# Attention pairs spread over three steps, with turned weights between a tile's input-side products

## The reference, cut to what matters

```python
scores = scale * q @ k.T                      # B=4, H=8, S=576, D=64, scale 1/8
scores = where(causal, -1e9, scores)
a = softmax(scores); local = a @ v
phi = where(q > 0, q, exp(q) - 1) + 1
mem_out = (phi @ M_prev) / (phi @ z_prev + 1e-6)
attn = g * mem_out + (1 - g) * local          # g = sigmoid(beta), one for each head
x = attn as 2304 tokens x 512
h = x @ w_in                                  # 512 x 1024
solu = h * softmax(h); ln = layernorm(solu) * g_ln
x = ln @ w_out                                # 1024 x 512
out = (sigmoid(x @ w_gate) * (x @ w_val)) @ w_out2    # d_ff 1536
```

## Time and profile before

| | |
|---|---|
| median of 3 runs | 964.6 us (963.66 to 966.36) |
| profiled execution | 962.04 us |
| its span | 960.3 us |
| TensorE busy | 907.2 us, 94% |
| VectorE, ScalarE, GpSimd busy | 408.5, 329.8, 183.5 us |
| mean granted TensorE clock | 0.979 |

### The profile page before, as it was taken

How to read it: one execution, slowest core, us unless ns; L and a number is a source line. 1 busy time by engine, 2 the same in 40 slices (tenths; PEclk the granted TensorE clock), 3 DMA queues, 4 the chain that set the end, 5 groups by cost and what they waited for, 6 DMA issues and landing times.

```text
span 960.3 us, 15231 instructions
## 1 busy us (share of the span) xinstructions
PE 907.2 (94%) x5584; PEld 749.3 (78%) x5584; DVE 408.5 (43%) x972; ACT 329.8 (34%) x740; POOL 183.5 (19%) x144
## 2 busy tenths in 40 slices
PE   5787789999999999999799999999999999999997
PEld 2555557777777777878699989989998998998997
DVE  5666776666766676354414422122112112112112
ACT  3455545545554555345524211121112112112111
POOL 4344322222222120125407410010001001001000
PEclk9889999999999999999999999999999999999999
DMA  5131111111111100400305000000000000000000
GB/s 155 49 127 41 51 40 38 31 33 38 38 38 38 38 26 14 132 1 1 99 1 165 0 33 1 1 18 15 0 0 33 0 0 33 0 0 33 0 0 33
DMA packets 36786, 33.51 MB, mean 35 GB/s; under 512 B 5776, under 2 KB 27280, under 8 KB 36752
## 3 DMA queue, kind: packets, MB, share of 16 engines
q1 hardware_dynamic: 36752, 33.06, 11.6%
HBM read 28.33 MB, written 4.72 MB: 34 GB/s over the span
## 4 chain that ended last, share of the span: by engine, by line
PE 87%; DVE 5%; issue 2%; POOL 2%; ACT 1%; DMA 1%; POOLq 0%; ACTq 0%; SPq 0%; DVEq 0%
PE m_bk L1066 8%; PE s_bk L1089 6%; PE tt_bk L1174 5%; PE s_bk L1176 5%; PE s_bk L1174 5%; PE s_bk L1175 5%; PE tt_bk L1176 5%; PE tt_bk L1175 5%; PE o_bk L1007 5%; PE tt_bk L999 4%; PE s_bk L953 4%; PE o_bk L1089 4%; PE m_bk L1191 3%; PE m_bk L1190 3%; PE m_bk L1189 3%; PE s_bk L1066 2%
## 5 line engine op out<-in xcount | busy, mean ns | idle before, releaser
L886 DVE TENSOR_TENSOR gv<-gv,s_bk 128x384 f32<-128x384 f32 x71 | 39.4, 554 | 289.4 <-PE s_bk L1176 289.4
L530 ACT ACTIVATE p_nat<-s_bk,negmax 128x512 f32<-128x512 f32 (+2 forms) x144 | 77.9, 548 | 94.9 <-DVE negmax L729 94.8
L597 ACT ACTIVATE gv<-tt_bk 128x384 f32<-128x384 f32 x70 | 34.5, 492 | 206.7 <-PE tt_bk L1176 206.7
L1174 PE MATMUL tt_bk<-x_hi,w_hi 128*128 128x384 f32 x280 | 94.7, 338 | 8.2 <-POOL x_lo L492 8.2
L1174 PE MATMUL s_bk<-x_hi,w_hi 128*128 128x384 f32 x288 | 96.3, 334 | 0.0
L1176 PE MATMUL s_bk<-x_hi,w_lo 128*128 128x384 f32 x288 | 96.2, 334 | 0.0
L1175 PE MATMUL s_bk<-x_lo,w_hi 128*128 128x384 f32 x288 | 96.2, 334 | 0.0
L1176 PE MATMUL tt_bk<-x_hi,w_lo 128*128 128x384 f32 x280 | 94.3, 337 | 0.0
L1175 PE MATMUL tt_bk<-x_lo,w_hi 128*128 128x384 f32 x280 | 94.0, 336 | 0.0
L604 ACT CAST gv_hi<-gv 128x384 fp32r<-128x384 f32 x72 | 36.9, 513 | 158.0 <-PE m_bk L1191 135.9
L729 DVE TENSOR_REDUCE negmax<-s_bk 128x1 f32<-128x512 f32 (+2 forms) x144 | 67.4, 515 | 51.0 <-PE s_bk L953 42.7
(11 more groups left out here) (144 smaller groups left out, 1846.6 us busy)
## 6 DMA issues: line engine op xcount, KB each, us to landing
qkT<-in_q SPq DMA_DIRECT2D x16, 288.0 KB, 2.8
qkT<-in_k SPq DMA_DIRECT2D x16, 288.0 KB, 2.8
out<-o_sb SPq DMA_DIRECT2D x18, 256.0 KB, 2.0
v_raw<-in_v SPq DMA_DIRECT2D x16, 256.0 KB, 2.7
w_raw<-in_moe_w_gate SPq DMA_DIRECT2D x12, 256.0 KB, 4.5
w_raw<-in_moe_w_val SPq DMA_DIRECT2D x12, 256.0 KB, 4.9
w_raw<-in_moe_w_out SPq DMA_DIRECT2D x12, 256.0 KB, 6.0
xT<-in_moe_w_in SPq DMA_DIRECT2D x1, 2048.0 KB, 8.5
```

Source lines behind the costliest of these rows:

```text
L530: nc.scalar.activation(dst, s_tile(tile), ACT.Exp, bias=negmax[:, n:n + 1], accum_out=den[:, n:n + 1]).then_inc(exp_ok, 1)
L1174: mm(o, w3_hi[f][:, a], x2_hi[:, d, :], start=d == 0, stop=False)
```

## The change

A pair now takes three steps: its scores and exponentials in step g, the rest of its normalization, its memory output and its turned weights in step g + 1, its weighted values in step g + 2. Turned weights stand between the blocks of the tile's input-side products, and the output products follow in two blocks around the tail tile's scores. `M0` becomes 6, so the last tile of the stage is in a seventeenth step without scores. The mask products go: VectorE adds a float32 mask to the scores, scales by -1/8, writes the sum to `p_nat` (now two buffers) and takes the minimum in one instruction; ScalarE exponentiates in place. q and k get second buffers and are loaded one step ahead; `qs` and `qmin` go. ScalarE makes `qrelu`, VectorE the feature (`feature`); GpSimd keeps only splits and the power. ScalarE copies five fills, VectorE two. The weighted values of the tail go to a bank of their own (`m_bk[0]`), in one function `weighted` that is `weighted_main` followed by `weighted_tail`, with the memory's five transposes first. Loops over steps are unrolled. Of new functions the whole is shown; the old functions of the same names are taken out.

```diff
-    ACT_FILLS = [n for n in range(NF) if n % 2 == 0]
-    DVE_FILLS = [n for n in range(NF) if n % 2 == 1]
+    ACT_FILLS = [0, 2, 4, 5, 6]
+    DVE_FILLS = [1, 3]
...
-    M0 = HP + 1
+    M0 = HP + 2
...
-    T_END = LAST - M0
+    T_END = PAIRS - M0
...
-        W1_AT = {0: (0, 1), 1: (2, 3)}
-        W2_AT = {2: (0, 1, 2), 3: (3, 4, 5), 4: (6, 7)}
+        W1_AT = {1: (0, 1), 2: (2, 3)}
+        W2_AT = {4: (0, 1), 5: (2, 3), 6: (4, 5, 6, 7)}
...
+            def step(g):
+                if g < LAST:
+                    wait(sp, s_ready, NU * g)
+                    wait(sp, qexp_ok, g)
+                    wait(sp, qrelu_ok, g)
+                    sp.wait_ge(q_in, 16 * g + 16)
+                    sp.wait_ge(k_in, 16 * g + 16)
+                    load_q(g + 1)
+                    load_k(g + 1)
+                if g > 1:
+                    sp.wait_ge(o_ready, 2 * g - 2)
+                    load_v(g - 1)
+                if 0 < g < PAIRS:
+                    sp.wait_ge(mem_ready, 2 * g)
+                    load_mz(g)
...
+            def step(g):
+                for c in W1_AT.get(g, ()):
+                    split_w1(c)
+                for f in W2_AT.get(g, ()):
+                    split_w2(f)
+                if g >= M0:
+                    rstd(g - M0)
+                if g >= M0 - 1:
+                    split_x(g - M0 + 1)
...
+            def feature_relu(g):
+                act.wait_ge(q_in, 16 * g + 16)
+                wait(act, phi_ok, g)
+                nc.scalar.activation(qrelu[:, :], qkT[:, g % 2, 0, :], ACT.Relu).then_inc(qrelu_ok, 1)
...
+            def exp_tile(g, n):
+                tile = order[n]
+                unit = [tile in u for u in UNITS].index(True)
+                act.wait_ge(max_ok, NU * g + unit + 1)
+                nc.scalar.activation(p_tile(g, tile), p_tile(g, tile), ACT.Exp, bias=negmax[:, n:n + 1], scale=-1.0,
+                                     accum_out=den[:, n:n + 1]).then_inc(exp_ok, 1)
...
+            def early_step(g):
+                exp_tile(g, 0)
+                exp_tile(g, 1)
+                if g > 1:
+                    keep_both(g - 2)
+                for n in range(2, 6):
+                    exp_tile(g, n)
+                if g:
+                    keep_pt(g - 1, 0)
+                    keep_pt(g - 1, 2)
+                exp_tile(g, 6)
+                exp_tile(g, 7)
+                if g:
+                    keep_pt(g - 1, 4)
+                    keep_pt(g - 1, 5)
+                    keep_pt(g - 1, 6)
+                feature_relu(g + 1)
+                exp_tile(g, 8)
+                feature_exp(g + 1)
+                for c in W1_AT.get(g, ()):
+                    split_w1(c)
+                for f in W2_AT.get(g, ()):
+                    split_w2(f)
...
+            def step(g, t):
+                if g < PAIRS:
+                    exp_tile(g, 0)
+                    exp_tile(g, 1)
+                if t:
+                    moe_ln(t - 1)
+                keep_both(g - 2)
+                if g < PAIRS:
+                    for n in range(2, 6):
+                        exp_tile(g, n)
+                keep_pt(g - 1, 0)
+                if g < PAIRS:
+                    exp_tile(g, 6)
+                    exp_tile(g, 7)
+                if g < LAST:
+                    feature_relu(g + 1)
+                keep_pt(g - 1, 2)
+                keep_pt(g - 1, 4)
+                keep_pt(g - 1, 5)
+                keep_pt(g - 1, 6)
+                moe_exp(t)
+                if g < PAIRS:
+                    exp_tile(g, 8)
+                moe_square(t)
+                for f in W2_AT.get(g, ()):
+                    split_w2(f)
+                moe_x(t + 1, x_done(t + 1))
+                if g < LAST:
+                    feature_exp(g + 1)
+                if t:
+                    moe_y(t - 1)
...
+            def unit_max(g, n):
+                if n == 0:
+                    wait(dve, pt_filled, NF * (g - 1))
+                dve.wait_ge(mask_ok, 3)
+                dve.wait_ge(s_ready, NU * g + n + 1)
+                for tile in UNITS[n]:
+                    c = order.index(tile)
+                    w = keys(tile)
+                    to, m = p_tile(g, tile), mask[:, FULL * P - min(w, FULL * P):FULL * P]
+                    if tile == TAIL_TILE:
+                        to = to.rearrange("p (a n) -> p a n", a=2)
+                        m = mask_tail[:, :].rearrange("p (a n) -> p a n", a=2)
+                    last = nc.vector.tensor_tensor_reduce(out=to, in0=s_tile(tile), in1=m, scale=-SCALE, scalar=3.0e38,
+                                                          op0=ALU.add, op1=ALU.min, accum_out=negmax[:, c:c + 1])
+                last.then_inc(max_ok, 1)
...
+            def feature(g):
+                dve.wait_ge(qrelu_ok, g + 1)
+                dve.wait_ge(qexp_ok, g + 1)
+                wait(dve, mem_ready, 2 * g)
+                nc.vector.scalar_tensor_tensor(out=phi[:, 0:S], in0=qexp[:, :], scalar=1.0, in1=qrelu[:, :], op0=ALU.min,
+                                               op1=ALU.add).then_inc(phi_ok, 1)
...
+            def early_step(g):
+                unit_max(g, 0)
+                unit_max(g, 1)
+                if g:
+                    normalize(g - 1, 1)
+                    normalize(g - 1, 2)
+                unit_max(g, 2)
+                unit_max(g, 3)
+                if g:
+                    scale_memory(g - 1, 0)
+                    scale_memory(g - 1, 1)
+                    keep_pt(g - 1, 1)
+                unit_max(g, 4)
+                unit_max(g, 5)
+                if g:
+                    keep_pt(g - 1, 3)
+                feature(g)
+                unit_max(g, 6)
+                normalize(g, 0)
+                for f in W2_AT.get(g, ()):
+                    scale_w2(f)
...
+            def step(g, t):
+                if g < PAIRS:
+                    unit_max(g, 0)
+                    unit_max(g, 1)
+                if t > 1:
+                    moe_store_x(t - 2)
+                normalize(g - 1, 1)
+                if t:
+                    moe_ln_low(t - 1)
+                normalize(g - 1, 2)
+                if g < PAIRS:
+                    unit_max(g, 2)
+                    unit_max(g, 3)
+                scale_memory(g - 1, 0)
+                scale_memory(g - 1, 1)
+                keep_pt(g - 1, 1)
+                if g < PAIRS:
+                    unit_max(g, 4)
+                    unit_max(g, 5)
+                keep_pt(g - 1, 3)
+                if g < PAIRS:
+                    feature(g)
+                    normalize(g, 0)
+                moe_max(t)
+                moe_rows(t)
+                moe_stats(t)
+                if g < PAIRS:
+                    unit_max(g, 6)
+                for f in W2_AT.get(g, ()):
+                    scale_w2(f)
+                moe_var(t)
+                moe_norm(t)
...
-            def score_mask(tile):
-                n = keys(tile)
-                mm(s_tile(tile)[:, n - P:n], ident_b[:, :], mask_t[:, :], start=True, stop=False, skip_group_check=True)
...
+            def copied(g, n):
+                if n in ACT_FILLS:
+                    pe.wait_ge(pt_act_ok, NA * g + ACT_FILLS.index(n) + 1)
+                else:
+                    pe.wait_ge(pt_dve_ok, ND * g + DVE_FILLS.index(n) + 1)
...
+            def early_step(g):
+                scores(g, 0)
+                if g > 1:
+                    weighted(g - 2)
+                scores(g, 1)
+                if g:
+                    memory(g - 1, None)
+                scores(g, 2)
+                if g:
+                    for n in range(5):
+                        turn_p(g - 1, n)
+                scores(g, 3)
+                if g:
+                    turn_p(g - 1, 5)
+                    turn_p(g - 1, 6)
...
+            def step(g, t):
+                if g < PAIRS:
+                    scores(g, 0)
+                if t > 1:
+                    moe_out_t(t - 2)
+                if t:
+                    pe.wait_ge(pt_act_ok, NA * (g - 1))
+                    pe.wait_ge(pt_dve_ok, ND * (g - 1))
+                    moe_transpose(t - 1)
+                weighted(g - 2)
+                wait(pe, yt_ok, t - 1)
+                if g < PAIRS:
+                    scores(g, 1)
+                memory(g - 1, t)
+                pe.wait_ge(x_ok, 2 * (g - 1))
+                wait(pe, u_ok, t)
+                moe_hidden(t, 0, 8)
+                turn_p(g - 1, 0)
+                turn_p(g - 1, 1)
+                moe_hidden(t, 8, 12)
+                if g < PAIRS:
+                    scores(g, 2)
+                moe_hidden(t, 12, 16)
+                turn_p(g - 1, 2)
+                turn_p(g - 1, 3)
+                moe_hidden(t, 16, 20)
+                turn_p(g - 1, 4)
+                turn_p(g - 1, 5)
+                moe_hidden(t, 20, 24)
+                turn_p(g - 1, 6)
+                if t:
+                    if g < PAIRS:
```

(92 more changed lines are left out.)

280 lines of the change are left out of this document (74 added, 206 removed).

## The result

The changed kernel takes **995.5 us** (median of 4 runs, 993.24 to 996.86), the kernel before 964.3 us beside it (4 runs, 963.66 to 966.36): a ratio of 1.0319, with a 95% interval of 1.0296 to 1.0341. It is slower, as forecast, but by 31 us where I had 8.4; the time lies outside my range of 955 to 988.

A forecast was written before the change was run, and what follows sets the result against it. TensorE fills the 25.45 us steady step, while waits set early steps. Tile 0 came 8.3 us sooner, but nine steps grew to 27.7 us, putting tile 11 8.2 us later: 973 us forecast, range 955 to 988.

The forecast's parts named there:

- Sign and bound: Whole kernel: slower, chance 0.70, because added waits make a steady step 27.7 us although TensorE's own work shrinks.
- TensorE's own sum: Steady step: TensorE alone would need 24.2 us instead of 25.45, with the mask products and some interruptions gone.
- (a): Steady step, first fill of turned weights: TensorE waits 0.2 us for the second half of the scaled memory.
- (b): Steady step, fifth fill: TensorE waits 1.84 us for ScalarE's copy of the third fill, queued behind relu and feature.
- (c): Steady step, the tile's transposes: TensorE waits 1.42 us for VectorE's scaling, which runs beside GpSimd's split of x.
- The maxima as products with a reduction: VectorE's score maxima: the new form costs nothing, at most 0.1 us each; 1.22 us against 1.22 for 1,024 columns.
- The early step: Steps before the steady stage: VectorE sets 14.5 us a step, plus 0.8 for the clock; step 6 begins near 91 us.
- From tile 0 to tile 9: Steady stage between those tiles' transposes: nine steps of 27.7 us less 1.8, from 124.5 to 372.0 us.
- The clock rival: Stretches of waits and transposes drop TensorE's clock in most steps, about 1.7 us each, 15 us in all: 988 us; chance 0.15.
- The larger early gain: Early steps overlap better and take 13.3 us, so six steps give 12 us more: 961 us; chance 0.13.
- The rival without waits: Steady steps without (b) and (c) take 24.4 us, ending 28 us before the forecast: 945 us; chance 0.12.

The follow-up runs named there:

- The first two experiments: Each against the changed kernel: ScalarE's relu moved behind its copies of turned weights, 975.49 us; the square moved ahead of the tail tile's exponential, 977.86 us.
- The fourth experiment: Changed kernel with GpSimd's weight splits delayed to the next step, behind its third score unit: 982.01 us, 1.0184 of the kernel before.
- the kernel with all edits: Changed kernel with relu late, square first, output rows before the next x, GpSimd's weight splits timed and its power first: 940.67 us, 0.9770 of the kernel before.
- the fifth: Changed kernel with delayed GpSimd weight splits, and tile 0's power and next x split ahead of the weight blocks: 980.19 us, 1.0172 of the kernel before.
- the second experiment: Changed kernel with ScalarE squaring the tile's rows before the tail tile's exponential: 977.86 us, 1.0141 of the kernel before.

## Why the prediction was off

**Sign and bound: right.** TensorE's own work did shrink, and the waits that the new order puts in took more than it gave. But the 31 us are not those of my sum: the steady waits are, the early part's are not.

**TensorE's own sum: right in kind, a little small.** I had 24.2 us a step. With nearly all waits gone it is 24.4 (24.67 less 0.26), and in the changed kernel, with four waits, 27.98 less 3.09 leaves 24.9. The difference is how a listed wait is counted: from the modelled end of the product before it, 0.39 us after that product's start, while in a full queue the next product starts 0.23 us after it (299.17 and 299.40, then the wait up to 301.53). So a wait costs TensorE 0.16 us beyond its listed length, which for the three that are gone makes the 0.5. I had priced none.

**Waits (a), (b), (c): right.** 0.22, 1.74 and 1.13 us against 0.2, 1.84 and 1.42. The unknown `feature` took 0.75, as scaled from the row of 384 columns; relu and the copy 0.68 and 0.57. For (c) the chain from the last fill's start held within 0.2 us: `moe_rows` 2.70 later (306.06), the square 3.43 after that instead of 3.25, and the transposes 10.20 after the fill instead of 10.10. I had let the output rows hold TensorE to a moment inside this wait, and they did. The first two experiments show (b) and (c) by taking them away.

**The maxima as products with a reduction: right.** By form, the largest form of the new line took 0.68 to 0.69 us for 512 columns and the tail's 0.76, where the plain maximum of the tail took 0.758.

**The early step: the step that failed.** The forecast had VectorE's work as "less some stretching by GpSimd, makes 11.4", then 14.5 and 0.8 for the clock, and step 6 near 91. The terms named there give 13.27 less 0.87 less 1.1 plus 0.75, which is 12.05, so the stretching stood in the sum as 0.65 taken off. At 14.70 the undisturbed step bears out the 14.5. The stretching was the term that was mis-sized, and had the wrong sign: it grew, to 4.3 us in steps 2 and 3. I used the very mechanism in wait (c), from the tile's scaling that took 1.55 instead of 0.81 beside a split, and didn't ask which instructions of VectorE the weight splits would now meet. They met the scalings in steps 2, 3 and 5 and cost the chain 2.12 + 2.16 twice and 1.73 once, 10.3 us. Step 6 began at 103.89, 12.9 us later than forecast; the other 2.6 are mostly the clock, which took more than my 0.8 a step in steps 2 and 3 (0.83 and 0.76; with the scalings free 1.00). Inside step 6 the scalings took 3.92 (2.8 too many), and its 37.43 us to tile 0's transposes against my 33.5 gave the other 3.9. The fourth experiment moved only GpSimd's splits and got 13.4 of the 16.8 us back. That GpSimd's weight blocks would hold tile 0's power was forecast rightly: it started 10.0 us after `moe_rows` (128.83 to 138.84), and I had 10.5.

**From tile 0 to tile 9: 6.8 us, in two parts.** 2.5 are nine times 0.28. The other 4.3 are the clock, but for 0.3: the first interval was 30.50 long (clock 0.91) and one of the others 29.82 (0.94), with a fifth fill's wait of 2.02 instead of 1.74. From tile 9 to tile 11's first product it was 2.9 us more, and that is the clock too: it fell around the transposes of tiles 9 and 10, which took 1.75 and 1.65 us. With relu moved it didn't fall there, and the same stretch took 26.56 us (376.59 to 403.15), for a forecast of 26.9.

**The clock rival: real in part, not what set the steady step.** Windows of the changed kernel: the waits and transposes around tile 5's, the same around tile 9's, and three windows around a fifth fill:

```profile
283.50:285.58 2.08, 0.94 (x8) 0.45 (x5) 1.85 (x4) 0.90 (x2) 1.39 (x2) 1.00 0.00 0
285.58:287.58 2.00, 2.00 (x17) 1.72 (x19) 1.93 (x8) 1.50 (x5) 0.00 (x0) 1.00 0.03 8
...
393.59:395.59 2.00, 0.66 (x5) 0.45 (x5) 1.86 (x4) 0.24 (x1) 1.30 (x2) 1.00 0.02 4
395.59:397.59 2.00, 2.00 (x11) 2.00 (x12) 1.93 (x8) 0.80 (x2) 0.00 (x0) 0.55 0.04 8
...
270.00:271.00 1.00, 0.00 (x0) 0.00 (x0) 0.93 (x4) 0.32 (x1) 0.00 (x0) 1.00 0.00 0
271.00:272.00 1.00, 0.02 (x1) 0.05 (x1) 0.50 (x2) 0.83 (x2) 0.00 (x0) 1.00 0.03 8
...
273.00:274.00 1.00, 1.00 (x4) 0.81 (x3) 0.00 (x0) 0.72 (x2) 0.00 (x0) 0.50 0.00 0
```

Around tile 5's transposes the clock stays at 2.4 GHz with TensorE busy for 0.94 of 2.08 us; so it does around those of tiles 1 to 8 (0.86 or 0.87 busy in the 2.00 us before each). Around tile 9's it fell to 1.2 GHz, after a stretch with 0.66 busy in 2.00 us, and around tile 10's likewise. The fall inside a steady step came behind a fifth fill, where TensorE had done nothing for 2.02 us. So the rival's fall around the transposes is real at two tiles, and not in most steps. Falls elsewhere cost more: with the first interval and the fall behind the fifth fill the clock took some 7 of the 9.7 us by which everything behind tile 0's transposes was late, where the rival had 15. (The fall near the middle of the kernel before does not show in the earlier trace rows, which I named for it; its trace has one, a mean of 0.57 from 476 to 484 us.) By the rule of the Trainium skill, "TensorE: Matmul & The Clock Gate", Part 4, that a PE-mode transpose doesn't count as busy for the clock as a product does, I had made a fall in most steps; the trace doesn't bear that consequence out.

**The other rivals.** The larger early gain didn't come: the early part was the one that got longer. The rival without waits, 945 us, is near what the kernel with all edits takes (940.7), in part by luck: its steady step would have been 24.4 us and is 24.67, and 6.4 us come from tile 0's transposes, at 118.06 where my sum has 124.5. The forecast said that it needed `feature` released before the fourth fill. It needed less: relu had only to stand behind the copies, and the square ahead of the tail tile's exponential.

**What stays open.** Why the clock falls in one step and not in another with the same waits. With the scalings free step 5 still had 0.80 in the fourth experiment and 1.00 in the fifth, steps 2 and 4 1.00 in the fourth and 0.89 in the fifth. The fifth fill's wait of 1.99 us in the second experiment was not followed by a fall, one of 2.02 in the changed kernel was. I can say what a fall cost in each place, not what called it.

## What to carry to other kernels

When work moves to another step, look at both engines that would run side by side there, not only at the sum of each: a GpSimd operation of 2.5 us cost VectorE nothing or 2.1 us, by which VectorE instruction it met. Before giving up a new order that is slower, take the waits that it added one by one; here a few calls moved within the queues of ScalarE and GpSimd turned 3.2% slower into 2.3% faster. The gain on the bounding engine (the masks, 9.1 us) I measured only in the kernel whose steady step has almost no wait; what it is worth beside the waits was not tested.

## What the runs showed of the hardware

- An in-SBUF scaling on VectorE and a two-input product of a few elements both stand still while a GpSimd product runs: 3.26 us for 1.14 and 2.32 for 0.16. It works the other way as well when VectorE is first: GpSimd's split took 1.82 for 1.27.
- A TensorE wait costs 0.16 us beyond its listed length, which counts from the modelled end of the product before: products of 512 columns that start 0.23 us apart are listed with 0.39 each. Three waits taken out of the step bear it out (0.5 us of other time gone).
- A standstill of 2.02 us was followed by 1.2 GHz from about 273 to 276 us, and its step was 1.84 us longer than its neighbours, 0.28 of it the longer wait. Waits of 1.71 to 1.74 us in the steps around it, and one of 1.99 in the second experiment (step 26.84 for 26.57), were not followed by a fall.
